# The opening of attention with two expert layers: head pairs first, masks copied by ScalarE, whole rows loaded, products read by nothing

## The reference

```python
scores = q @ k.T / 8                      # per head
mask = (pos_q // 64) >= (pos_k // 64)     # whole blocks of 64
attn = softmax(where(mask, scores, -1e9)) # sum + 1e-9 in the divisor
x = (attn @ v), heads side by side        # 2304 x 512
for w_in, w_out, a in ((moe, 1.0), (moe2, 1.702)):
    h = x @ w_in
    x = (h * sigmoid(a * h)) @ w_out
```

## Time and profile before

| | |
|---|---|
| median of 3 runs | 948.2 us (948.01 to 948.34) |
| the profiled execution | 947.78 us |
| its span, first to last instruction | 946.0 us |
| mean granted clock of TensorE | 1.000 |
| TensorE busy | 928.8 us, 98% |
| VectorE, ScalarE, GpSimd busy | 528.2, 384.5, 299.6 us |

### The profile page before, as it was taken

How to read it: one execution, slowest core, us unless ns; L and a number is a source line. 1 busy time by engine, 2 the same in 40 slices (tenths; PEclk the granted TensorE clock), 3 DMA queues, 4 the chain that set the end, 5 groups by cost and what they waited for, 6 DMA issues and landing times.

```text
span 946.0 us, 14419 instructions
## 1 busy us (share of the span) xinstructions
PE 928.8 (98%) x5304; PEld 795.0 (84%) x5304; DVE 528.2 (56%) x1096; ACT 384.5 (41%) x854; POOL 299.6 (32%) x408
## 2 busy tenths in 40 slices
PE   5999999999999999999999999999999999999998
PEld 4888877787778777877788889999999999999997
DVE  6777756565657556655445435454654455644443
ACT  4677634453435434543323323232433233523222
POOL 6899337653554354435717200000000000000000
PEclk9999999999999999999999999999999999999999
DMA  9555695795788764888537986434364534364431
GB/s 267 168 149 159 184 315 175 232 326 179 220 268 263 245 195 137 267 268 272 181 116 279 360 314 210 125 111 131 104 191 110 134 102 132 107 195 104 131 102 67
DMA packets 65190, 179.57 MB, mean 190 GB/s; under 512 B 7136, under 2 KB 8800, under 8 KB 59232
## 3 DMA queue, kind: packets, MB, share of 16 engines
q1 hardware_dynamic: 64688, 177.99, 59.8%
q10 hardware_dynamic: 432, 0.66, 0.2%
HBM read 130.02 MB, written 44.56 MB: 185 GB/s over the span
## 4 chain that ended last, share of the span: by engine, by line
PE 94%; DVE 1%; POOL 1%; ACT 1%; issue 0%; POOLq 0%
PE ps_y L967 20%; PE ps_y L1025 13%; PE ps_a L1026 7%; PE ps_h L950 7%; PE ps_h L952 6%; PE ps_h L951 6%; PE ps_a L929 5%; PE ps_a L917 4%; PE ps_a L998 4%; PE ps_a L1001 4%; PE ps_a L1000 4%; PE ps_h L998 3%; PE ps_h L1001 3%; PE ps_h L1000 3%; PE ps_a L869 2%; PE ps_a L897 2%
## 5 line engine op out<-in xcount | busy, mean ns | idle before, releaser
L967 PE MATMUL ps_y<-g_hi,w_hl 128*128 128x512 f32 (+1 forms) x640 | 189.1, 378 | 0.0
L1025 PE MATMUL ps_y<-o_hi,w_out 128*128 128x512 f32 x368 | 139.9, 391 | 0.0
L967 PEld LDWEIGHTS ps_y<-g_hi,w_hl 128*128 128x128 f32 x640 | 112.0, 189 | 16.6 <-DVE g_lo L1376 0.4
L967 PE MATMUL ps_y<-g_lo,w_hl 128*128 128x512 f32 (+1 forms) x320 | 118.5, 370 | 0.0
L1152 ACT ACTIVATE g_f<-ps_h 128x512 f32<-128x512 f32 (+1 forms) x71 | 40.8, 575 | 189.2 <-PE ps_h L952 189.2
L950 PE MATMUL ps_h<-x_hi,w_hl 128*128 128x512 f32 (+1 forms) x284 | 111.6, 393 | 0.2 <-POOL w_hl L750 0.2
L1371 DVE SCALAR_TENSOR_TENSOR g_f<-g_f,ps_h 128x512 f32<-128x512 f32 x63 | 43.3, 688 | 117.8 <-ACT g_f L1152 117.4
L952 PE MATMUL ps_h<-x_lo,w_hl 128*128 128x512 f32 (+1 forms) x284 | 107.7, 379 | 0.0
L951 PE MATMUL ps_h<-x_hi,w_hl 128*128 128x512 f32 (+1 forms) x284 | 107.2, 377 | 0.0
L1026 PE MATMUL ps_a<-o_hi,w_out 128*128 128x256 f32 x368 | 103.0, 280 | 0.0
L1133 ACT ACTIVATE p_sb<-ps_a,nmax 128x512 f32<-128x512 f32 (+4 forms) x128 | 72.3, 572 | 67.0 <-DVE nmax L1340 66.5
(11 more groups left out here) (151 smaller groups left out, 1899.3 us busy)
## 6 DMA issues: line engine op xcount, KB each, us to landing
w_form<-f_split SPq DMA_DIRECT2D x168, 256.0 KB, 2.7
w_hl<-w_split SPq DMA_DIRECT2D x30, 1024.0 KB, 7.5
w_raw<-w_chunks SPq DMA_DIRECT2D x42, 512.0 KB, 5.7
w_split<-w_hl SPq DMA_DIRECT2D x16, 1024.0 KB, 7.8
f_split<-stage SPq DMA_DIRECT2D x24, 512.0 KB, 5.7
o_split<-stage SPq DMA_DIRECT2D x16, 512.0 KB, 4.1
w_out<-o_split SPq DMA_DIRECT2D x16, 512.0 KB, 7.5
k_raw<-kT SPq DMA_DIRECT2D x28, 288.0 KB, 5.9
```

The lines of the kernel that those rows point to most:

```text
L967: last = nc.tensor.matmul(bank_y(t, k), lhs, rhs, start=(part == 0 and f == 0 and (t > 0 or k % 2 == 0)), stop=(part == 2 and f == NF - 1) ...
L1025: nc.tensor.matmul(y_main(k), lhs, rhs[:, h, 0:512], start=begin, stop=end, skip_group_check=True)
```

## The change

The arrays of the first block are laid out with head pairs outermost, so that group 0 holds the slices k = 0 and 1 of all batches and group 1 holds 2 and 3. The inputs still come in two halves of 512 columns. The splits become four of 256 columns, two for each group; TensorE runs values 0 ahead of transposes 1, and the transposes write to banks 0 and 1. ScalarE's and VectorE's orders change accordingly.

Six products of the identity with itself, whose result is read by nothing, stand ahead of the first scores, and six behind the second ones.

The masks' factors are put in place by four copies on ScalarE ahead of its first exponential, and no longer by four DMAs on SyncE's queue. The value load of the first blocks is issued behind the first queries. GpSimd's last piece of chunk 0 no longer waits for the first normalised group (`s_enm`). Queries and keys are laid out so that a row of the tile, both heads, is one run of memory. An inversion adds 1e-9 to both rows' sums in one instruction.

```diff
-EG = E0 // 2
+GROUPS = 2
+EG = E0 // GROUPS
+EJ = JOBS // GROUPS
+WARM = (6, 6)
...
 def e_cols(part, g):
...
+def e_halves(part, m):
+    return part[:, E0 // 2 * m:E0 // 2 * (m + 1)]
...
 def e_stat(part, g):
-    return part[:, JOBS // 2 * g:JOBS // 2 * (g + 1)]
-def e_out(e):
-    return bank(2) if e == 0 else ps_y[:, 0:512]
-def e_by_batch(e):
-    return e_out(e).rearrange("p (b k c) -> p b k c", b=B, c=BLK)
-def e_tile(part, e):
-    return part[:, e:NK:2, 0:B * BLK].rearrange("p k (b c) -> p b k c", c=BLK)
+    return part[:, EJ * g:EJ * (g + 1)]
+def e_score(g):
+    return ps_y[:, 512 * g:512 * g + EG]
+def e_out(m, e):
+    if m == 0:
+        return bank(2)[:, 0:EG // 2] if e == 0 else ps_h[:, 0:EG // 2]
+    return ps_y[:, 512 * e:512 * e + EG // 2]
+def e_by_batch(m, e):
+    return e_out(m, e).rearrange("p (k b c) -> p k b c", k=NK // 2, c=BLK)
+def e_tile(part, m, e):
+    x = part[:, NK // 2 * m:NK // 2 * (m + 1), 0:B * BLK].rearrange("p k (b c) -> p k b c", c=BLK)
+    return x[:, :, e::2, :]
...
-            sp.dma_start(raw(n)[0][D * half:D * half + D, :, :],
-                         qT[n, :, :].rearrange("(h d) c -> d h c", h=2)).then_inc(s_q[n % 2], 16)
+            sp.dma_start(raw(n)[0][D * half:D * half + D, :, :].rearrange("d h c -> d (h c)"),
+                         qT[n, :, :]).then_inc(s_q[n % 2], 16)
...
-            sp.dma_start(raw(n)[1][D * half:D * half + D, :, :],
-                         kT[n, :, :].rearrange("(h d) c -> d h c", h=2)).then_inc(s_k[n % 2], 16)
+            sp.dma_start(raw(n)[1][D * half:D * half + D, :, :].rearrange("d h c -> d (h c)"),
+                         kT[n, :, :]).then_inc(s_k[n % 2], 16)
     def copy_keys(n):
...
-    def place_masks():
-        sp.wait_ge(s_mask, 8)
-        for h in range(2):
-            sp.dma_start(q_mask[D:P, h, :].bitcast(F32), mask_q[D:P, :]).then_inc(s_maskd, 16)
-            sp.dma_start(k_mask[D:P, h, :].bitcast(F32), mask_k[D:P, :]).then_inc(s_maskd, 16)
...
-        sp.dma_start(e_cols(q0_raw, g), e_cols(q0T, g)).then_inc(s_eq[g], 16)
+        sp.dma_start(e_halves(q0_raw, g), e_halves(q0T, g)).then_inc(s_eq[g], 16)
...
+    load_queries(0)
...
-    load_queries(0)
...
-    place_masks()
...
-            if i == 0 and j == PIECES - 1:
-                pool.wait_ge(s_enm, 1)
...
 def _(pe):
+    def warm(n):
+        for _ in range(n):
+            nc.tensor.matmul(bank(2)[:, 0:P], ident[:, :], ident[:, :], start=True, stop=True, skip_group_check=True)
     def early_scores(g):
...
-        for i in range(JOBS // 2):
+        for i in range(EJ):
...
-                last = nc.tensor.matmul(ps_y[d, 512 * g + BLK * i:512 * g + BLK * i + BLK],
+                last = nc.tensor.matmul(e_score(g)[d, BLK * i:BLK * i + BLK],
...
     def early_transposes(g):
...
-        for i in range(JOBS // 4):
-            last = nc.tensor.transpose(ps_y[:, 512 * (2 + g) + P * i:512 * (2 + g) + P * i + P],
+        for i in range(EJ // 2):
+            last = nc.tensor.transpose(bank(g)[:, P * i:P * i + P],
...
-        for s in range(JOBS // 4 * g, JOBS // 4 * (g + 1)):
+        for j in range(EJ // 2):
+            s = EJ // 2 * g + j
+            col = BLK * j
...
-                    last = nc.tensor.matmul(e_out(e)[d, BLK * s:BLK * s + BLK], v0_sb[keys, s, d], pt0[keys, s, d],
+                    last = nc.tensor.matmul(e_out(g, e)[d, col:col + BLK], v0_sb[keys, s, d], pt0[keys, s, d],
...
-                pe.wait_ge(s_maskd, 64)
+                pe.wait_ge(s_maskd, 4)
...
-            pe.wait_ge(s_exl, 2)
+            pe.wait_ge(s_exl, 4)
...
-            pe.wait_ge(s_exl, 1 + k % 2)
+            pe.wait_ge(s_exl, 2 * (k // 2 + 1))
...
-    early_scores(0)
-    early_scores(1)
...
+    warm(WARM[0])
+    for g in range(GROUPS):
+        early_scores(g)
+    warm(WARM[1])
...
+    early_values(0)
...
-    early_values(0)
...
     def early_take(g):
...
-        nc.scalar.activation(pt0[:, JOBS // 4 * g:JOBS // 4 * (g + 1), :],
-                             ps_y[:, 512 * (2 + g):512 * (3 + g)].rearrange("p (s c) -> p s c", c=P),
-                             ACT.Copy).then_inc(s_etk, 1)
-    def early_split(e):
+        nc.scalar.activation(pt0[:, EJ // 2 * g:EJ // 2 * (g + 1), :],
+                             bank(g)[:, 0:EG].rearrange("p (s c) -> p s c", c=P), ACT.Copy).then_inc(s_etk, 1)
+    def early_split(m, e):
...
-            act.wait_ge(s_epv, 2)
-        nc.scalar.activation(e_tile(x_hi0, e), e_by_batch(e), ACT.Copy).then_inc(s_exh, 1)
+            act.wait_ge(s_epv, m + 1)
+        nc.scalar.activation(e_tile(x_hi0, m, e), e_by_batch(m, e), ACT.Copy).then_inc(s_exh, 1)
+    def place_masks():
+        act.wait_ge(s_mask, 8)
+        for h in range(2):
+            nc.scalar.activation(q_mask[D:P, h, :], mask_q[D:P, :], ACT.Copy).then_inc(s_maskd, 1)
+            nc.scalar.activation(k_mask[D:P, h, :], mask_k[D:P, :], ACT.Copy).then_inc(s_maskd, 1)
...
-        act.dma_start(e_cols(k0_raw, g), e_cols(k0T, g)).then_inc(s_ek[g], 16)
+        act.dma_start(e_halves(k0_raw, g), e_halves(k0T, g)).then_inc(s_ek[g], 16)
+    place_masks()
...
-    queries_end(0)
...
+    early_split(0, 0)
+    early_split(0, 1)
...
+    queries_end(0)
...
-    early_split(0)
-    early_split(1)
+    early_split(1, 0)
+    early_split(1, 1)
...
     def early_multiply(g):
...
-                                e_stat(e_rden, g).unsqueeze(2).to_broadcast([P, JOBS // 2, BLK]),
+                                e_stat(e_rden, g).unsqueeze(2).to_broadcast([P, EJ, BLK]),
...
-    def early_split(e):
-        dve.wait_ge(s_exh, e + 1)
-        nc.vector.tensor_tensor(e_tile(x_lo0, e), e_by_batch(e), e_tile(x_hi0, e).bitcast(F32),
+    def early_split(m, e):
+        dve.wait_ge(s_exh, 2 * m + e + 1)
+        nc.vector.tensor_tensor(e_tile(x_lo0, m, e), e_by_batch(m, e), e_tile(x_hi0, m, e).bitcast(F32),
...
     def invert(n, u):
...
-        nc.vector.tensor_scalar(den_e[:, a:a + 1], den[:, a:a + 1], 1e-9, None, ALU.add)
-        nc.vector.tensor_scalar(den_e[:, b:b + 1], den[:, b:b + 1], 1e-9, None, ALU.add).then_inc(s_den, 1)
+        nc.vector.tensor_scalar(den_e[:, a:b + 1], den[:, a:b + 1], 1e-9, None, ALU.add).then_inc(s_den, 1)
...
+    early_split(0, 0)
+    early_split(0, 1)
...
+    early_split(1, 0)
+    early_split(1, 1)
...
-    early_split(0)
-    early_split(1)
...
     def heads_first(a):
...
+    def pairs_first(a):
+return a.reshape(B, NK, *a.shape[1:]).swapaxes(0, 1).reshape(JOBS, *a.shape[1:])
+    def by_depth(a):
+return a.reshape(JOBS, 2, D, -1).transpose(0, 2, 1, 3).reshape(JOBS, D, -1)
...
-"q0T": qp[:, :, :BLK].transpose(1, 0, 2).reshape(P, E0),
-"k0T": kp[:, :, :BLK].transpose(1, 0, 2).reshape(P, E0),
-"v0": vp[:, :BLK].reshape(JOBS // 2, P, P).transpose(1, 0, 2).reshape(P, JOBS // 2 * P),
-"qT": qp[:, :, BLK:],
-"kT": kp,
+"q0T": pairs_first(qp[:, :, :BLK]).transpose(1, 0, 2).reshape(P, E0),
+"k0T": pairs_first(kp[:, :, :BLK]).transpose(1, 0, 2).reshape(P, E0),
+"v0": pairs_first(vp[:, :BLK]).reshape(JOBS // 2, P, P).transpose(1, 0, 2).reshape(P, JOBS // 2 * P),
+"qT": by_depth(qp[:, :, BLK:]),
+"kT": by_depth(kp),
```

6 lines of the change are left out of this document (3 added, 3 removed).

## The result

The changed kernel takes 950.31 us (median of 7 runs, 949.99 to 952.39), the kernel before took 948.2 beside it (947.42 to 948.4). The ratio is 1.0027, 95% interval 1.0018 to 1.0037: slower by 0.27%, or 2.5 us (2.1 by the medians). The forecast was 947.2 and no measurable change, the range ended at 949.0: wrong in sign and size.

A forecast was written before the change was run, and what follows sets the result against it. Bound: the attention chain up to row maxima at 18.95, and GpSimd's weight chunks. Gains 0.20 + 0.50 + 0.17 + 0.14 = 1.01 us from 947.78 gave 946.8; with 0.42 for the median, 947.2; range 945.4 to 949.0.

The forecast's parts named there:

- Step 6: Inversions: one addition less in each gains 0.07 us on each of two on the path, 0.14; bounds 0 and 0.3.
- Step 1: Opening: twelve unread products are hidden and raise TensorE's clock by T; one group's transposes take 0.60 us instead of 1.09.
- T: Start of the first transposes in the opening, 12.24 us in the kernel before; forecast not to move.
- Step 2: Opening's new order: row maxima at T + 6.5 us instead of T + 6.71; gain 0.2, bounds -0.1 and +0.3.
- Step 4: Both heads in one row: shorter load issue nearly ends the 0.52 us wait at 96.72; gain 0.50, bounds 0 and 0.52.
- Step 5: GpSimd's chunk chain runs 1.1 us or more earlier, ending TensorE's 0.17 us wait at 39.60; bounds 0 and 0.17.
- The end moves with the row maxima at 18.95: Bound claimed for the opening: exponentials follow job 0's row maxima, and each masked unit waits for the exponentials before it.
- VectorE is stretched beside a GpSimd that doesn't pause: Rival: three VectorE operations on the path each take 0.37 us longer, 1.1 in all, giving 948.3; chance 0.05.
- the clock is up already in the scores: Rival: the first six products raise the clock, T comes about 1.15 us earlier, giving 946.0; chance 0.22.
- the low clock: Rival: clock low through the opening, row maxima 1.6 us late, 949.0; decides once take 1 starts after T + 3.35; chance 0.13.
- Step 3: Masks copied by ScalarE from 4.76 to 7.1 us, hidden ahead of the first exponential at 8.45 with 1.3 to spare.

The follow-up runs named there:

- e11: Filled kernel (e5) with one addition of two columns in each inversion instead of two single ones: 949.52 us, ratio 1.0011.
- e10: Filled kernel (e5) with 6 unread products ahead of the scores instead of 9, and 19 behind them instead of 16: 947.62 us, ratio 0.9987.
- e2: Changed kernel with the inversion's addition again as two of one column: 950.66 us, ratio 1.0015.
- e5: Changed kernel with two additions and more unread products in TensorE's opening gaps (9 ahead of the scores, 16 behind, others later): 947.61 us, ratio 0.9990.
- e4: Kernel before with only the twelve unread products added, six ahead of the scores and six behind: 950.17 us, ratio 1.0012.
- e17: Changed kernel with two additions, and GpSimd's second weight chunk made to wait for the values of group 1: 949.66 us, ratio 1.0015.
- e14: Filled kernel with 6 and 19 products and two additions (e10), with the early blocks' values loaded ahead of the queries: 947.23 us, ratio 0.9979.
- e3: Kernel before with the merged addition as its only edit: 949.65 us, ratio 1.0006.
- e7: Kernel before with only the layout of both heads of queries and keys in one row: 947.86 us, ratio 0.9996.
- e15: Changed kernel with two additions and 2 and 8 unread products ahead of the second and third masked units: 949.92 us, ratio 1.0010.
- e8: Kernel before with both heads in one row and masks copied by ScalarE instead of four DMAs: 949.1 us, ratio 1.0004.

## Why the prediction was wrong, point by point

**What failed, in short.** The prediction added 1.01 us of gains; the kernel lost 2.5. Two of its terms fail by the runs. Step 6, a gain of 0.14 for the merged addition, is a loss of 1.9 us with the clock up (e11 against e10) and of about 1 in the changed kernel (e2). Step 1, "clock up at T and stays", failed in its second half: the clock fell at 13 us, and the kernel that has two additions and its gaps filled (e5) has a ratio of 0.9990 where e2 has 1.0015, 2.4 us less. With both put right the kernel is 0.9 us faster than before, near the forecast; that is partly luck, since steps 2 and 4 did not hold there either. Step 5 failed in its mechanism, as told below, but no run prices it alone.

**What bounds the kernel.** "The end moves with the row maxima at 18.95" was not enough. What the end follows is the key remainder of job 1, which is the later of two chains: ScalarE's key copy, behind the exponentials of unit 2 (in ten traces the remainder starts 3.71 to 3.94 us after the third row maxima), and GpSimd's chunks before it. From the remainder to job 4's end scores it takes 65.2 to 67.2 us in all twenty traces, which is a spread as wide as the loss itself, and from there to the end 848.98 to 849.84 in all but one, e4. The prediction had both chains. It even named the remainder's wait for ScalarE's key copies, but took those copies to stay where they were; it did not see that a delay of unit 2 moves them, and with them GpSimd.

**Step 5**, the gain from an earlier GpSimd, turned round in the profile. Before, the 1.53 us in which GpSimd stood for a chunk were the time in which VectorE's multiply took 0.89 us. The change gave GpSimd its loads earlier, as forecast (fourth chunk at 25.04 instead of 26.67; the 0.17 at 39.60 is gone), and VectorE's multiplies took 0.35 and 0.82 longer, on the chain that then decided. That this lost time on the whole is argued from the two profiles, not shown: e17 shortened the multiplies again and was no faster. The rival "VectorE is stretched beside a GpSimd that doesn't pause" had the mechanism, with 1.1 us of price, but looked for it ahead of the row maxima, and gave it 0.05. There, too, it occurred: the products of rows took 0.92 and 0.86 us for 0.69.

**Step 1.** The products are hidden, and T came 0.97 earlier, near the 1.15 of the rival "the clock is up already in the scores". "Clock up at T and stays" failed: the granted clock was 1.00 at T and 0.50 from 13 to 19.5, after idle stretches of 2.35 and 0.78 us. Both rivals were true, one after the other: the row maxima came 0.97 earlier by T and 1.17 later behind it.

**Step 2.** The row maxima came at T + 7.88 instead of T + 6.5, bound by the end scores at 1.2 GHz and not by VectorE. Take 1 started at T + 3.71, past the stated point of T + 3.35 from which the low clock decides. In e14, with the clock up, it is T + 6.92: the forecast's order was 0.4 too short even then.

**Step 3** held: masks from 4.79 to 6.86, the first exponential at 7.93, one table load.

**Step 4** failed: 0.50 forecast, nothing shown. The 0.33 us of a plain chunk, taken from the earlier trace rows, is not the price of these rows; the issue is 1.11. The wait at the end scores follows the landing of the load, 5.6 to 7.4 us from issue to copy in twenty traces, with no order by kind of row. It is gone in the first profile, in which TensorE came later itself, and is 1.75 us in the second.

**Step 6** had the wrong sign: 0.14 gain forecast, 0.32 lost behind the first row maxima, 0.47 at 119.93, and 0.6 to 1.9 us by e2, e3 and e11. From job 4's end scores to the end all seven traces with one addition take 849.69 to 849.84 us, and eleven of thirteen with two 848.98 to 849.35 (the others are e7, 849.67, unexplained, and e4 with its late fall of the clock).

The Trainium skill has a rule that fits steps 5 and 6. By VectorE: DVE Perf Modes, Mode 2×_2P, a fp32 operation with one source, in SBUF on both sides, reads its first and second half through two ports at once if its outermost dimension can be halved; and GPSIMD Engine Reference, 1. Specifications, says that GpSimd shares VectorE's SBUF interfaces, with contention for such operations and for those with two SBUF inputs. The traces agree: 128x2 and the multiplies are stretched, the 128x1 has nothing to halve and isn't, and the differences of 128x256 that read PSUM took 0.40 to 0.43 us everywhere. That it is the ports, no run here shows; they show only who is stretched and beside what. The size, 1.04 us for two columns, is told by the runs alone.

What stays open: why GpSimd's second chunk starts later in the filled kernels (15.7 to 16.5, for 14.9 to 15.7 in the changed kernel's others, but for the two in which the early values were late as well), which is what puts the multiplies beside the copies there; what sets the landing of job 4's queries; where the kernel before loses 1.7 us in half of its executions; and how much of e14's gain is clock and how much phase. By its trace against e15's, two additions in both: 1.43 us at the first row maxima (18.49 for 19.92), 1.14 behind them.

## What to carry to other kernels

When an engine that shares something with the critical one is set free earlier, look up what the critical one did in the idle time that disappears: here a multiply of VectorE took 0.8 us less while GpSimd stood idle for 1.5. Merging two small operations saves nothing if the merged one belongs to a class that contends; compare the maximum of its durations beside the other engine, not the median. Before you believe a cost seen in one profile, follow it to the next point where two chains meet: most of the low clock near 26 was absorbed there, and a gain of 0.7 at 18.95 was too. And look at the clock of every execution, not only of the profiled one: a kernel whose executions fall in two kinds needs many of them before a change of 0.2% can be priced.

## What the runs showed of the hardware

TensorE's clock rose to 2.4 GHz during the scores when products had run ahead of them (in e4 as well). Without products it rose behind the second transposes, but for e8, where the last scores were already faster (234 ns at the shortest for 311) and the clock was 0.50 again from 12 to 18 us. In the changed kernel it fell to 0.50 after 2.35 and 0.78 us of idleness with 0.65 of work between. A wait of 2.21 was followed by 0.50 in one profile, and one of 2.35, in the same kernel, by 1.00: whether a wait costs the clock can't be told from its length. In the kernel before, 51 executions with a mean clock of 1.000 had a median of 947.9 us, and 37 with 0.998 one of 949.5. An addition of 128x2 on VectorE beside GpSimd took up to 1.049 us, at its shortest 0.155, and the three followed above ended 0.02 or 0.03 us behind a GpSimd instruction. Products read by nothing can hold back real work: 9 of them, 4.21 us at 1.2 GHz, moved the scores from 4.79 to 5.66. And loads of the opening land up to 2 us apart from one execution to the next: the early values, issued behind the queries, took 8.0 to 10.1 us from issue.
